# A window attention and two feed-forward layers in one kernel: one unit's work put ahead of two copies, three exponentials moved, and a softmax moved into the wait for the halo

## The reference

```python
# attention over the last 7 tokens, with 8 heads of 24 features
w = exp(weight_gen - max(weight_gen, axis=-1))       # (2, 4096, 8, 7)
w = w / (sum(w, axis=-1) + 1e-09)
x = einsum('bshk,bskhg->bshg', w, last_7_tokens(x))  # -> (8192, 192)
# two feed-forward layers, 192 -> 2048 -> 192
h = x @ moe_w_in
x = (h * cos(h)) @ moe_w_out
h = x @ moe2_w_in
out = maximum(0.01 * h, h) @ moe2_w_out
```

## Time and profile before

| | |
|---|---|
| median of three runs | 1150.26 us |
| profiled execution, own time | 1151.76 us |
| its span, first to last instruction | 1150.0 us |
| PE busy | 1132.5 us (98% of the span) |
| DVE busy | 934.6 us (81%) |
| ACT busy | 724.9 us (63%) |
| POOL busy | 87.1 us (8%) |
| mean granted TensorE clock | 0.997 |

### The profile page before, as it was taken

The page is one execution under the profiler, slowest core; times in us unless marked ns, Lnnn a source line. Parts: engine busy times, 40 slices in busy tenths (PEclk is TensorE's granted clock), DMA queues, the critical chain, the costliest instruction groups (busy, mean ns, idle before and its releaser), DMA issues.

```text
span 1150.0 us, 22937 instructions
## 1 busy us (share of the span) xinstructions
PE 1132.5 (98%) x9766; PEld 996.1 (87%) x9766; DVE 934.6 (81%) x913; ACT 724.9 (63%) x775; POOL 87.1 (8%) x80
## 2 busy tenths in 40 slices
PE   7999999999999999999999999999999999999998
PEld 5778989988888888899998989988888898898976
DVE  7989798888979889697896978969798796978543
ACT  5666774766747666575665757566575665757544
POOL 5870000000000000000000000000000000000000
PEclk9999999999999999999999999999999999999999
DMA  9760201103011020201102011020201102010001
GB/s 257 203 129 1 63 2 32 45 1 77 1 37 41 1 76 1 54 24 31 47 1 76 1 36 42 4 74 1 47 31 30 48 1 77 1 37 7 1 15 29
DMA packets 85262, 48.41 MB, mean 42 GB/s; under 512 B 58156, under 2 KB 78762, under 8 KB 84776
## 3 DMA queue, kind: packets, MB, share of 16 engines
q1 hardware_dynamic: 80712, 41.70, 14.1%
q0 software_dynamic: 4448, 5.24, 2.5%
HBM read 35.12 MB, written 11.80 MB: 41 GB/s over the span
## 4 chain that ended last, share of the span: by engine, by line
PE 89%; DVE 4%; ACT 1%; issue 1%; ACTq 0%; DVEq 0%
PE slot L1200 41%; PE acc_a L1200 28%; PE acc_b L1200 18%; DVE g_lo L919 1%; DVE prods L327 0%; DVE prods L318 0%; ACT g_hi L732 0%; DVE gate L1017 0%; PE acc_b L1173 0%; ACT gate L795 0%; ACT L855 0%; PE acc_b L1174 0%; PE acc_a L1166 0%; PE acc_a L1165 0%; ACT taps_w L855 0%
## 5 line engine op out<-in xcount | busy, mean ns | idle before, releaser
L1200 PE MATMUL acc_a<-g_hi,out_hi_lo 64*128 64x512 f32 x2000 | 699.0, 390 | 0.0
L919 DVE TENSOR_TENSOR g_lo<-gate,g_hi 128x1024 fp32r<-128x1024 f32 x252 | 309.2, 1227 | 119.0 <-ACT g_hi L732 118.5
L1200 PE MATMUL acc_b<-g_hi,out_hi_lo 64*128 64x512 f32 x1000 | 389.6, 390 | 5.7 <-DVE g_lo L919 3.0
L1200 PEld LDWEIGHTS acc_a<-g_hi,out_hi_lo 64*128 64x128 f32 x2000 | 370.0, 185 | 26.6
L1200 PE MATMUL acc_a<-g_lo,out_hi_lo 64*128 64x512 f32 x1000 | 387.9, 388 | 0.0
L1200 PE MATMUL acc_b<-g_lo,out_hi_lo 64*128 64x512 f32 x1000 | 387.6, 388 | 0.0
L732 ACT ACTIVATE g_hi<-gate 128x1024 fp32r<-128x1024 f32 x252 | 267.3, 1061 | 97.4 <-PE acc_b L1200 78.0
L1200 PE MATMUL slot<-x_a_hi,in_a_lo 64*128 64x512 f32 x1024 | 301.8, 390 | 1.3 <-DVE g_lo L919 0.6
L1200 PE MATMUL slot<-x_a_lo,in_a_hi 64*128 64x512 f32 x1024 | 300.9, 388 | 0.4 <-DVE x_a_lo L938 0.4
L1200 PE MATMUL slot<-x_b,in_b_hi 64*128 64x512 f32 x1024 | 300.9, 388 | 0.2 <-DVE x_b L941 0.2
L1200 PE MATMUL slot<-x_a_hi,in_a_hi 64*128 64x512 f32 x1024 | 300.7, 388 | 0.0
(11 more groups left out here) (110 smaller groups left out, 1023.0 us busy)
## 6 DMA issues: line engine op xcount, KB each, us to landing
x_win<-in_x SPq DMA_DIRECT2D x14, 960.0 KB, 4.7
x_columns<-prods SPq DMA_DIRECT2D x56, 96.0 KB, 2.0
out<-turned_a SPq DMA_DIRECT2D x240, 16.0 KB, 1.5
x_raw_a<-x_columns SPq DMA_DIRECT2D x14, 256.0 KB, 2.8
out<-turned_b SPq DMA_DIRECT2D x120, 16.0 KB, 1.5
result<-x_columns SPq DMA_DIRECT2D x14, 128.0 KB, 3.0
out_raw<-in_moe_w_out SPq DMA_DIRECT2D x3, 512.0 KB, 8.6
out_hi_lo<-in_moe_w_out POOLq DMA_DIRECT2D x2, 768.0 KB, 10.7
```

The costliest lines, as they stand in the source:

```text
L919: nc.vector.tensor_tensor(g_lo[:, q % 2, :], result_of(i - b, q), g_hi[:, q % 2, :].bitcast(FP32), ALU.subtract)\
L1200: return nc.tensor.matmul(to, w[rows, :], x[rows, :], start=start, stop=stop)
```

## The change

The order of the work on DVE and ACT changes at five places, and one DMA issue and one wait move with it. No arithmetic is added or left out; POOL and PE keep their instructions.

- **Chunk 1's first unit.** The tail of softmax 2 moves from step 9 of iteration 0 to step 0 of iteration 1, behind the fraction of unit (1, 0) and ahead of its product. The product, `g_hi` and `g_lo` of unit (1, 0) are done in step 0 of iteration 1: on ACT ahead of the copy `mid_a`, on DVE the product ahead of `fold` and `mid_b`, and `g_lo` right behind them.
- **POOL's wait.** The low parts of the second layer's weights no longer wait for softmax 2's tail but for `g_lo` of unit (1, 0).
- **The later softmax.** The exponentials move from step 10 to step 13 and the sine's table from step 12 to step 14; heads stand together after step 12 (before: steps 8, or 13 and 14), tails at steps 16 and 17 (before: 13, 14 and 16).
- **The second softmax of the prologue.** Its load moves from SP's queue to ACT's. Its head on DVE moves from behind the first attention to the place where DVE waits for the halo rows; its exponential moves to the beginning of ACT's queue, ahead of the weight copies.
- **The first split.** ACT's `split_high` of chunk 0 moves ahead of the last two weight copies, and DVE's sum, guard and invert of softmax 1 ahead of `split_low`.

```diff
-        EXP_STEP, SINE_STEP = 10, 12
+        EXP_STEP, SINE_STEP = 13, 14
...
-        SOFT_AT = {(0, 9): [(2, part) for part in TAIL_PARTS]}
+        SOFT_AT = {}
         for n, (begin, end) in enumerate(((1, 1), (2, 3), (4, 5)), 2):
-            SOFT_AT[begin, 8 if n == 2 else 13] = [(n, "max")]
-            SOFT_AT.setdefault((begin, 8 if n == 2 else 14), []).append((n, "subtract"))
-            SOFT_AT[end, 13] = [(n + 1, "sum")]
-            SOFT_AT[end, 14] = [(n + 1, "guard"), (n + 1, "invert")]
-            SOFT_AT[end, 16] = [(n + 1, "multiply")]
+            SOFT_AT[begin, 12] = [(n, "max"), (n, "subtract")]
+            SOFT_AT[end, INPUT_STEP] = [(n + 1, "sum"), (n + 1, "guard"), (n + 1, "invert")]
+            SOFT_AT[end, INPUT_STEP + 1] = [(n + 1, "multiply")]
...
             load_columns(0)
-            load_gen(1)
             load_columns(1)
...
-            pool.wait_ge(soft, soft_count(2, "multiply"))
+            pool.wait_ge(lo_ready, unit(1, 0) + 1)
...
+                if (i, step) == (1, 0):
+                    high_part(1, 0)
                 j = first_out(i, step)
...
+                if n == len(HI_PIECES) - 1:
+                    split_high(-1, INPUT_STEP, 0)
                 nc.scalar.activation(b_lows(W1.in_b_lo_raw, cols), b_pairs(W1.in_b_raw, cols), ACT.Copy,
                                      scale=PER_TURN).then_inc(w1_raw, 1)
...
             exponentials(0)
+            act.dma_start(taps_w[:, HEAD_ROWS[1], :], gen_rows[:, HEAD_ROWS[1], :])\
+                .then_inc(gen_loaded[1], 16)
+            exponentials(1)
             act.wait_ge(padded, 2)
...
-            split_high(-1, INPUT_STEP, 0)
-            exponentials(1)
             act.wait_ge(ident_ready, 2)
...
                 pending_low(i, step)
+                if (i, step) == (1, 0):
+                    for part in TAIL_PARTS:
+                        softmax(2, part)
+                    product(1, 0)
                 j = first_out(i, step)
...
+                if (i, step) == (1, 0):
+                    low_part(1, 0)
...
-            for instruction in attention(0, dve):
+            first, *others = attention(0, dve)
+            first()
+            for part in HEAD_PARTS:
+                softmax(1, part)
+            for instruction in others:
                 instruction()
```

More of the change, by code:

```diff
@@ L736, in pending_high @@
                 b, prev = back(step, 1)
-                if is_unit(i - b, prev):
+                if (i, step) != (1, 1) and is_unit(i - b, prev):
                     high_part(i - b, UNITS.index(prev))
@@ L903, in _, with product, low_part @@
         def _(dve):
+            def product(i, q):
+                slot = slots[UNITS[q] % SLOTS][:, :, :].rearrange("p a n -> p (a n)")
+                dve.wait_ge(cos_ready, first_units(i, q))
+                nc.vector.scalar_tensor_tensor(result_of(i, q), slot, RADIANS, gate[:, q % 2, :],
+                                               ALU.mult, ALU.mult).then_inc(g_ready, 1)
+            def low_part(i, q):
+                dve.wait_ge(hi_ready, unit(i, q) + 1)
+                nc.vector.tensor_tensor(g_lo[:, q % 2, :], result_of(i, q),
+                                        g_hi[:, q % 2, :].bitcast(FP32), ALU.subtract)\
+                    .then_inc(lo_ready, 1)
             def pending_low(i, step):
                 b, prev = back(step, 1)
-                if is_unit(i - b, prev):
+                if (i, step) != (1, 1) and is_unit(i - b, prev):
                     q = UNITS.index(prev)
@@ L917, in pending_low @@
                         return
[L918 to L921, removed]
+                    low_part(i - b, q)
             def split_low(step, chunk):
@@ L1040, in step_of @@
                             .then_inc(done, 1)
[L1041 to L1045, removed]
+                elif in_first and (i, step) != (1, 0):
+                    product(i, q)
+                if (i, step) == (1, 0):
+                    low_part(1, 0)
                 if i < LAST:
@@ L1092, in _ @@
                 nc.vector.tensor_tensor(lo, raw, hi, ALU.subtract).then_inc(w1_first_lo, 1)
-            for part in HEAD_PARTS:
+            for part in TAIL_PARTS[:-1]:
                 softmax(1, part)
             split_low(INPUT_STEP, 0)
-            for part in TAIL_PARTS:
-                softmax(1, part)
+            softmax(1, TAIL_PARTS[-1])
             of_chunk_1 = list(attention(1, dve))
```

## The result

The changed kernel takes 1155.1 us (median of six runs, 1154.4 to 1155.5), the kernel before 1150.28 in runs on the same chip: a ratio of 1.0038, 95% interval [1.0029, 1.0048]. It is 4.8 us slower. I had forecast 1150.3, which is no change. The profiled execution took 1155.07 with a span of 1153.3, 3.3 more than the span of before.

What follows compares the result with a forecast made beforehand. PE, busy for 98% of the span, was taken to bound the kernel. 3.0 + 0.9 + 1.4 - 5.2 + 0 = 0.1 gained, called 0: profiled 1151.8, forecast 1150.3 us (chance 0.42), range 1146.6 to 1154.6.

Steps and rivals of the forecast that it cites:

- Unit (1, 0): Start of iteration 1: 0.4 us of PE waiting in place of 3.67 lost, clock stays up, PE ahead by 3.1.
- POOL gets in first: Rival, unit (1, 1): `g_lo` waits for POOL's third weight instruction, 4.5 us lost, time 1154.2; chance 0.22.
- The units behind it: After unit (1, 1): POOL's last nine instructions may hold up a `g_lo` by another 0.1 us.
- `mid_b`: Iteration 1: softmax 2's head leaves DVE's queue ahead of `fold`, PE's 0.71 us wait and restart go, 0.9 gained.
- Iterations 3 and 5: PE's 0.38 us waits for `g_lo` go with the exponentials moved out of step 10; 0.7 each, 1.4 gained.
- The splits: Ends of iterations 1, 3 and 5: split products come late, PE waits, 1.2 + 2.0 + 2.0 = 5.2 us lost.
- The prologue: Before iteration 0: taken as 0, with bounds of 0.7 us gained and 1.7 lost.
- I take 8.7, between them: Prologue: landing time assumed for the second softmax's load, between an early landing and 10.3; attention then ends 1.05 us later.
- x_a_hi starts at 20.8 as before: Prologue: ACT's first split starts no later, although the attention ends 1.05 us later.
- PE's first long wait: Prologue: ended by a `g_lo` shut out by a POOL product; half a microsecond on DVE was to move nothing, 0.
- The rival on a late load: Prologue: the load is late and DVE's chain passes POOL's, 1.7 us lost, time 1152.0; chance 0.10.
- The runs lie 1.5 below it: Whole kernel: step from the profiled execution, 1151.8, to the forecast run time, 1150.3 us.

Runs made afterwards that it cites:

- second profile of before: The kernel before the change, unchanged, profiled once more: 1150.09 us, with a span of 1148.3.
- the kernel with the head at step 12: Kernel before with the unit (1, 0) part and, in iteration 1 only, the later head, exponential, reload (after step 17) and tail: 1147.54 us, ratio 0.9978.
- the late reload: The changed kernel with the sine's table loaded again after step 17 instead of step 14: 1150.03 us, ratio 0.9997.

## Why the prediction was wrong, step by step

- **Unit (1, 0): right.** 3.10 was gained for 3.1. `g_lo` of unit (1, 1) asked at 77.79 and was let in ahead of POOL's third instruction, which took 3.38 instead of 2.39; the wait was 0.30 for 0.4. "POOL gets in first" did not happen, nor in any of the other seven profiles with POOL's new wait (0.28 to 0.30 each). The forecast margin of 0.1 was 0.15 to 0.18 in all eight: POOL's start and DVE's request both follow from the same `g_lo`, so it was no toss of a coin.
- **The units behind it: too small.** I gave POOL's last nine instructions 0.1. Two collisions in a row at 88 to 92 cost 0.65. I had looked at the first unit behind POOL's start and not at all those up to its end.
- **`mid_b`: wrong, in size and in kind.** The forecast was 0.9 for the head's move. Its 1.70 us left the queue, but the same change had brought PE forward by 2.4, and a DVE that is busy for 19.90 of 20.00 us (88 to 108 in the changed kernel) does not come forward with it. I worked out each step against the trace of before, where PE was not yet early. The two belong together: unit (1, 0) alone gains nothing (1150.34), with the head moved it gains 2.6 (1147.54).
- **Iterations 3 and 5: right.** 1.37 was gained for 1.4.
- **The splits: right.** 4.83 was lost for 5.2, by the mechanism named, waits on `x_a_lo` and `x_b` at the ends of iterations 1, 3 and 5. The run with the reload behind them gave back 5.1.
- **The prologue: the step that failed.** It stands in the sum as "I take 0 for the prologue", and it cost 1.6 against the profile that I used and 2.6 on average. The mistake has three parts. The first is "I take 8.7, between them": the load landed at 10.24, at the upper bound of 10.3, 6.6 us after its issue on ACT's queue (at 3.63, not 4.05) as against 6.3 on SP's. I chose the middle where the nearest row, for the same bytes, said 6.3. The halo part was then 2.56 late, which I had priced as 2.7. The second is "x_a_hi starts at 20.8 as before": that cover, ACT's weight copies, was the property of one execution. In the second profile of before ACT is idle for 0.84 us at that place, and in the five other kernels with this prologue the copies hold `x_a_hi` back by some 0.4 us at most; there was nothing for the delay to hide behind. The third is that PE's first long wait would not follow, as long as the load sets POOL's time. POOL's two products did stay where they were (the second ended at 34.56 and now at 34.41), but the wait went from 33.26 to 35.06, since `g_lo` then asked at 32.93 and met the second product instead of the first, for 2.02. The rival on a late load (1.7 lost, 1152.0) named this mechanism. Its price fits the profile that it was made from (1.6) and not the average (2.6).
- **From the profile to the median.** "The runs lie 1.5 below it" was true of the profile of before and is not true of the changed kernel, whose profiled execution (1155.07) is its median. This alone put the forecast 1.5 too low. The late prologue of that one profile explains 0.8 of it, by the mean of the seven; the rest stays open.

In sum, between the two profiles 3.3 us were lost where a gain of 0.1 was forecast. 0 became 1.6 in the prologue, 0.9 gained became 0.05 at `mid_b`, and 0.1 became 0.65 behind unit (1, 1). That is 3.0. The splits were 0.4 cheaper than forecast, and 0.8 are the drift to the end and the small ones between. The other 1.5 of the 4.8 is the step from the profile to the median.

The rule that I weighed from the Trainium skill ("DMA: Bandwidth & Descriptors", "Queues, rings and completion order") has each DMA engine take turns between its queues, and I drew from it that a second queue adds no bandwidth and that the halo rows come later. The trace agrees with the first for the load itself: it took 6.6 us on ACT's queue and 6.3 on SP's, and over all thirteen profiles 6.2 to 7.3 on ACT's and 5.1 to 6.3 on SP's. What I drew for the halo rows was wrong: they were there by 8.79 with the load on ACT's queue, and by 8.14 or earlier in the run with the head behind the halo products, where DVE had waited for them until 8.88 before.

One thing was not run: the head at its new place with the load still on SP's queue. So how much of the prologue's loss the new queue itself makes, against the head's place, is not shown.

## What to carry to other kernels

A gain at one place is worked out again at the next place that the same engine feeds: ask how busy that engine is between the two (19.87 of 20.00 us with the part on unit (1, 0) alone), because a full queue turns PE's lead into the next wait. Work that is put into "idle time" costs its own length and the wait for its input, in a chain that has no room behind it. And cover that one execution shows (an engine that happens to be late anyway) is looked up in a second execution before a step is priced at nothing.

## What the runs showed of the hardware

- **The clock after idle time.** In the changed kernel the granted clock fell to 0.50, the 1.2 GHz level, behind PE's wait of 2.21 at 35.06. In the kernel with the head at step 12 PE waited 2.18 at the same place, and the windows view right behind it has 1.00. This is the changed kernel:

```profile
35.10:38.40 3.30, 3.30 (x16) 2.83 (x18) 3.30 (x3) 1.06 (x1) 3.30 (x4) 0.50 1.16 266
```

Then the kernel with the head at step 12:

```profile
32.70:36.10 3.40, 3.40 (x30) 3.02 (x32) 3.40 (x4) 1.21 (x2) 3.40 (x3) 1.00 0.99 347
```

  With the late reload the wait was 2.59 and the clock stayed up as well, while behind the waits of 1.77 and 1.80 at unit (1, 0) it fell in both profiles of before. No wait of up to 1.54 us was followed by a fall in any profile from 22 us on; among those of 1.76 to 2.59 both happen (2.50 with a fall, 2.59 without). The length of the idle time alone does not tell; what does stays open.
- **The port.** A DVE subtraction on SBUF that asks while POOL's runs of back-to-back subtractions go on was let in between two of them in each of these rows, and it was POOL's next that grew (3.38 for 2.39, 5.90 for 4.78 in two). DVE never waited for more than the POOL instruction that was running, in these rows and in all thirteen profiles from 22 us on.
